# A kernel of sparse attention and two MLPs: the splitting jobs of its first 17 slots dealt out anew

## The reference

```python
scores = scale * np.matmul(q, k.transpose(0, 1, 3, 2))
kth = np.partition(scores, -top_k, axis=-1)[..., -top_k:-top_k + 1]      # top_k = 32
scores = np.where(scores >= kth, scores, -1000000000.0)
attn = softmax(scores)
out = np.matmul(attn, v)
```

```python
h = x @ w_in                                             # MLP 1
g = np.where(h >= 1, h, np.where(h <= -1, 0.0, (h + 1) ** 2 / 4))
x = g @ w_out
h = np.maximum(x @ w_in2, 0.0)                           # MLP 2
out = h * h @ w_out2
```

## Time and profile before

| | us |
|---|---|
| median of 3 runs | 1287.52 (1285.49 to 1288.41) |
| the profiled execution, whole | 1287.39 |
| its span, first to last instruction | 1285.6 |
| PE busy | 1194.8 (93%) |
| DVE busy | 910.6 (71%) |
| POOL busy | 783.9 (61%) |
| ACT busy | 721.8 (56%) |

### The profile page before, as it was taken

One profiled execution on the slowest core, in us unless ns is written; L12 is line 12 of the kernel. 1 busy time (PEld: TensorE's weight loads), 2 busy tenths in 40 slices (PEclk: granted clock), 3 DMA queues, 4 the chain that ended last, 5 costly groups with the idle time before them and its releaser, 6 DMA issues.

```text
span 1285.6 us, 24517 instructions
## 1 busy us (share of the span) xinstructions
PE 1194.8 (93%) x8760; PEld 1132.5 (88%) x8760; DVE 910.6 (71%) x2039; ACT 721.8 (56%) x1617; POOL 783.9 (61%) x637
## 2 busy tenths in 40 slices
PE   2677888999999999999999999999999999999998
PEld 1566878988888999999999999999989999999997
DVE  5789899989899998989999999989861111111121
ACT  4555566766655476776767654556543565643332
POOL 2999787787788776777766767666562222222222
PEclk9966799999999999999999999999999999999999
DMA  5899748565879972543437851445429500780000
GB/s 194 275 341 349 255 164 274 187 232 209 321 254 341 387 300 74 170 166 122 130 114 263 314 197 39 140 151 198 147 77 354 217 34 1 265 325 8 27 17 17
DMA packets 98728, 245.89 MB, mean 191 GB/s; under 512 B 7344, under 2 KB 48304, under 8 KB 86320
## 3 DMA queue, kind: packets, MB, share of 16 engines
q1 hardware_dynamic: 98608, 244.33, 53.7%
HBM read 167.23 MB, written 77.07 MB: 190 GB/s over the span
## 4 chain that ended last, share of the span: by engine, by line
PE 69%; POOL 11%; ACT 8%; DVE 5%; issue 4%; DMA 1%; SPq 0%; ACTq 0%; POOLq 0%
PE h_ps L581 21%; PE y_ps L602 14%; PE y_ps L596 12%; PE pv_ps L540 6%; PE score_ps L581 6%; POOL s_sb L1045 4%; PE tr_ps L513 4%; POOL prob L1050 3%; PE score_ps L478 3%; DVE top L860 2%; DVE rest L862 2%; ACT prob L699 1%; POOL kq_lo L1029 1%; POOL w_out L1037 1%; ACT s_sb L676 1%
## 5 line engine op out<-in xcount | busy, mean ns | idle before, releaser
L1063 POOL TENSOR_TENSOR g_lo<-g_sb,g_hi 128x256 fp32r<-128x256 f32 x288 | 217.2, 754 | 405.1 <-ACT g_hi L778 404.9
L581 PE MATMUL h_ps<-xt_hi,w_in 128*128 128x256 f32 x1880 | 391.3, 291 | 3.5 <-DVE xt_lo L908 2.0
L581 PEld LDWEIGHTS h_ps<-xt_hi,w_in 128*128 128x128 f32 x1880 | 309.6, 191 | 6.7 <-issue 3.0
L860 DVE MAX8 top<-rest 128x8 f32<-128x576 f32 x432 | 303.8, 744 | 0.0
L1045 POOL TENSOR_SCALAR s_sb<-s_sb,top 128x576 f32<-128x576 f32 x144 | 258.4, 1794 | 51.5 <-DVE top L860 50.6
L581 PE MATMUL h_ps<-xt_lo,w_in 128*128 128x256 f32 x940 | 266.2, 283 | 0.0
L596 PE MATMUL y_ps<-g_hi,w_out 128*128 128x256 f32 x1152 | 232.6, 285 | 0.4 <-POOL g_lo L1063 0.3
L778 ACT ACTIVATE g_hi<-g_sb 128x256 fp32r<-128x256 f32 x288 | 121.0, 420 | 184.7 <-DVE g_sb L917 68.8
L862 DVE MATCH_REPLACE8 rest<-top,rest 128x576 f32<-128x576 f32 x288 | 211.4, 741 | 0.0
L602 PE MATMUL y_ps<-w_out,g_hi 128*128 128x512 f32 x576 | 203.3, 394 | 0.3 <-POOL g_lo L1063 0.3
L596 PEld LDWEIGHTS y_ps<-g_hi,w_out 128*128 128x128 f32 x1152 | 190.4, 193 | 1.7 <-POOL g_lo L1063 0.5
(11 more groups left out here) (79 smaller groups left out, 1954.9 us busy)
## 6 DMA issues: line engine op xcount, KB each, us to landing
w_in<-w_scratch SPq DMA_DIRECT2D x32, 1024.0 KB, 6.7
w_out<-w_scratch SPq DMA_DIRECT2D x32, 1024.0 KB, 8.0
ks<-ks_scratch SPq DMA_DIRECT2D x47, 576.0 KB, 5.5
qs<-qs_scratch SPq DMA_DIRECT2D x78, 256.0 KB, 4.4
stage<-in_w_dram SPq DMA_DIRECT2D x32, 512.0 KB, 4.7
w_scratch<-w_in SPq DMA_DIRECT2D x16, 1024.0 KB, 6.8
w_scratch<-w_out SPq DMA_DIRECT2D x16, 1024.0 KB, 8.3
v_sb<-in_vv_dram SPq DMA_DIRECT2D x48, 325.0 KB, 5.5
```

The costliest lines, as they stand in the source:

```text
L581: last = pe.matmul(h_bank(k), wi[:, f // 2, w, m, cols], x[:, m, :], start=(m == 0 and n == 0), stop=(m == KT - 1 and n == 2))
L860: dve.max(best, src[:, :]).then_inc(rank_step, 1)
L1063: pool.tensor_tensor(g_lo[k % 2][:, :], g_sb[k % 2][:, :], g_hi[k % 2][:, :].bitcast(F32), ALU.subtract).then_inc(g_lo_done, 1)
```

## The change

- Jobs in slots 0 to 18: no slot before 14 but slot 0 holds more than one splitting job on POOL. Preps 1 to 8 go from slots 0, 2, 4, 7, 9, 13, 15, 17 to slots 1, 3, 5, 11, 13, 17, 19, 29; preps 9 to 11 go from 28, 30, 32 to 31, 33, 35. Weight blocks 0 to 15 go to the slots of `W1_SLOT`; blocks 12 and 14 are split by DVE, in slots 14 and 15.
- Blocks 0 to 15 have four staging buffers: `xr` and `ys`, which are idle until slot 18, join the two. Three blocks are loaded before slot 0.
- `kq_scratch` holds whole rows of 1216 elements: `restack` has three DMAs (608, 608 and 320 KB) in place of six (two of 288 and four of 320 KB), and `load_qs` has two with pieces of 512 bytes in place of one with pieces of 1024.
- `restack` stands first in SP's slot, ahead of the loads of ks, v and qs.
- `split_first` is cut in two, and DVE ranks the first tiles between its parts; prep 0's subtraction goes from DVE to POOL.
- On DVE the sums of slot n-2 are handled one or two ranking steps later.
- `split_w` on POOL and DVE waits for the lo part of block i-2.

```diff
-PREP_SLOT = (-1, 0, 2, 4, 7, 9, 13, 15, 17, 28, 30, 32, 38, 41, 44, 47)
+PREP_SLOT = (-1, 1, 3, 5, 11, 13, 17, 19, 29, 31, 33, 35, 38, 41, 44, 47)
-W1_PER_SLOT = (1, 2, 1, 2, 1, 2, 1, 1, 1, 1, 1, 1, 1)
+W1_SLOT = [-1, 0, 0, 2, 4, 6, 7, 8, 9, 10, 12, 14, 14, 15, 15, 16]
+STAGE_SLOT = [-1, -1, -1, 0, 1, 2] + [s - 1 for s in W_SLOT[6:]]
...
 def by_vector(i):
-    return i >= WBLOCKS and i % 2 == 1
+    return i in (12, 14) or (i >= WBLOCKS and i % 2 == 1)
+def stage_at(i):
+    return i % 4 if i < WBLOCKS else i % 2
...
-    ks_dram = [scratch(f"ks_scratch{g}", [2, 2 * DIM, SEQ]) for g in range(PREPS)]
-    qs_dram = [scratch(f"qs_scratch{g}", [QT, 2, 2 * DIM, 2, P]) for g in range(PREPS)]
+    kq_dram = [scratch(f"kq_scratch{g}", [3, 2 * DIM, KQ]) for g in range(PREPS)]
...
+        def stage_of(i):
+            return (stage[0], stage[1], xr, ys)[stage_at(i)]
...
                 for x, part in enumerate((kq_hi, kq_lo)):
-                    sp.dma_start(ks_dram[g][x, :, :], part[:, 0:SEQ].bitcast(F32)).then_inc(restacked, 16)
-                    for var in range(2):
-                        sp.dma_start(qs_dram[g][:, x if var == 0 else 1 - x, :, var, :]
-                                     .rearrange("t p n -> p t n"),
-                                     part[:, SEQ:KQ].rearrange("p (t n) -> p t n", t=QT)
-                                     .bitcast(F32)).then_inc(restacked, 16)
+                    sp.dma_start(kq_dram[g][x, :, :], part[:, :].bitcast(F32)).then_inc(restacked, 16)
+                sp.dma_start(kq_dram[g][2, :, SEQ:KQ], kq_hi[:, SEQ:KQ].bitcast(F32)).then_inc(restacked, 16)
...
             def load_qs(g, t, i):
-                sp.dma_start(qs[i][:, :, :, :].bitcast(F32),
-                             qs_dram[g][t].rearrange("x (d h) v n -> (x d) h v n", h=2)).then_inc(qs_loaded[i], 16)
+                cols = slice(SEQ + P * t, SEQ + P * (t + 1))
+                for var in range(2):
+                    sp.dma_start(qs[i][:, :, var, :].bitcast(F32),
+                                 kq_dram[g][var:var + 2, :, cols].rearrange("x (d h) n -> (x d) h n", h=2)
+                                 ).then_inc(qs_loaded[i], 16)
...
             def slot(n):                        # SP
+                if n and n - 1 in PREP_SLOT:
+                    restack(PREP_SLOT.index(n - 1))
                 if n < NORMAL and n % 2 == 0:
                     if n // 2 + 1 < NORMAL // 2:
                         load_slot_ks(n // 2 + 1)
...
-                if n and n - 1 in PREP_SLOT:
-                    restack(PREP_SLOT.index(n - 1))
...
-            stage_block(0)
+            for i in range(3):
+                stage_block(i)
             restack(0)
-            load_kq(1)
...
-            split_first(0)                      # ACT
-            split_first(1)
+            split_first(0, 0)
+            split_first(1, 0)
             copy_scores(0, 0)
+            split_first(0, 1)
             copy_scores(0, 1)
-            split_kq(0)
+            split_first(1, 1)
+            split_new(-1)
...
                 both(0)                         # DVE, slot(n)
+                if n == 0:
+                    split_first(0, 1)
+                    split_first(1, 1)
...
-                if past:
-                    add_to_total(n - 2)
                 both(1)
...
-                if past:
-                    invert_total(n - 2)
-                both(2)
-                if past:
+                behind = 1 if n < UP_POS[0] // 3 else 0
+                for op in (2, 3, 4):
+                    if past and op == 2 + behind:
+                        add_to_total(n - 2)
+                    if past and op == 3 + behind:
+                        invert_total(n - 2)
+                    if op == 4:
+                        if past and not behind:
+                            scale_pv(n - 2)
+                        at(3 * n + 1)
+                    both(op)
+                if past and behind:
                     scale_pv(n - 2)
...
+            split_kq(0)                         # POOL, ahead of slot 0
+            for i in new_blocks(-1):
+                split_w(i)
```

More of the change, by code:

```diff
@@ L221, in build @@
         zeroed = sem("zeroed")
-        w_staged = [sem(f"w_staged{i}") for i in range(2)]
+        w_staged = [sem(f"w_staged{i}") for i in range(4)]
         first_loaded = [sem(f"first_loaded{i}") for i in range(2)]
@@ L646, in _, with split_first @@
         def _(act):
-            def split_first(t):
+            def split_first(t, a):
                 act.wait_ge(first_loaded[t], 16)
[L650 to L655, removed]
+                if a == 0:
+                    act.activation(ks[0][:, t, :], first_k(t), ACT.Copy).then_inc(first_hi, 1)
+                for var in range(2):
+                    rows = slice(DIM * var, DIM * (var + 1))
+                    act.activation(qs[a][rows, t, var, :], first_q(t, a)[rows, :],
+                                   ACT.Copy).then_inc(first_hi, 1)
             def split_kq(g):
@@ L659, in split_kq @@
                 if g:
-                    act.wait_ge(restacked, 16 * 6 * g)
+                    act.wait_ge(restacked, 16 * 3 * g)
                 act.activation(kq_hi[:, :], kq_lo[:, :].bitcast(F32), ACT.Copy).then_inc(kq_hi_done, 1)
@@ L939, in clear_corners, with split_first @@
                         dve.memset(prob[n % 2][rows, col:col + TAIL], 0.0).then_inc(zeroed, 1)
[L941 to L952, removed]
-                    dve.wait_ge(first_hi, 5 * t + 3 + 2 * a)
-                    for var in range(2):
-                        rows = slice(DIM * var, DIM * (var + 1))
-                        dve.tensor_tensor(qs[a][rows, t, 1 - var, :], first_q(t, a)[rows, :],
-                                          qs[a][rows, t, var, :].bitcast(F32),
-                                          ALU.subtract).then_inc(first_lo, 1)
+            def split_first(t, a):
+                if a == 0:
+                    dve.wait_ge(first_hi, 3 * t + 1)
+                    low = slice(DIM, P)
+                    dve.tensor_tensor(ks[0][low, t, :], first_k(t)[low, :], ks[0][low, t, :].bitcast(F32),
+                                      ALU.subtract).then_inc(first_lo, 1)
+                dve.wait_ge(first_hi, 3 * t + 3 if a == 0 else 8 + 2 * t)
+                for var in range(2):
+                    rows = slice(DIM * var, DIM * (var + 1))
+                    dve.tensor_tensor(qs[a][rows, t, 1 - var, :], first_q(t, a)[rows, :],
+                                      qs[a][rows, t, var, :].bitcast(F32),
+                                      ALU.subtract).then_inc(first_lo, 1)
             def split_w(i):
@@ L1014, in slot @@
                     scale_pv(n - 1)
-            split_first(0)
-            split_first(1)
-            split_kq(0)
+            split_first(0, 0)
+            split_first(1, 0)
             for n in range(SLOTS + 2):
@@ L1064, in lo_at, with new_blocks @@
                                        ALU.subtract).then_inc(g_lo_done, 1)
+            def new_blocks(n):
+                return [i for i in range(2 * WBLOCKS) if W_SLOT[i] == n and not by_vector(i)]
             def slot(n):
@@ L1077, in slot @@
                     split_kq(PREP_SLOT.index(n))
-                for i in range(2 * WBLOCKS):
-                    if W_SLOT[i] == n:
-                        split_w(i)
+                for i in new_blocks(n):
+                    split_w(i)
             pool.memset(ident[:, :], 0.0).then_inc(constants_set, 1)
```

44 lines of the change are left out of this document (25 added, 19 removed).

## The result

Forecast 1275.1 us (1268 to 1283). Measured: a median of 1289.61 us over 20 executions (1287.20 to 1295.30), with 1287.28 for the kernel before on the same chips (20 executions, 1285.49 to 1288.98). The ratio is 1.002 (95% interval 1.0012 to 1.0028): no gain, and probably a loss of 0.2%.

A forecast was written before the change was run, and what follows sets the result against it. PE was taken to bound the kernel from about 400 us on, carrying savings in the POOL- and DVE-limited front to the end. A gain of 17.5 less 5.2 is 12.3 from 1287.39: 1275.1 us, range 1268 to 1283.

The forecast's parts named there:

- The start and slots 2 to 9: Earlier first mask, then DVE setting every slot at 10.07 us: slot 10 reached 19.0 us earlier, taken as 17.5.
- rival A: Front bound by data, with slots 3 to 9 longer and the first ks load late: 1284.9 us, chance 0.12.
- Slots 10 to 19: Jobs land where there were none and lengthen the chain: 5.2 us given back, ends 0 and 9.5.
- Slots 20 on: Preps 8 to 11 move later but stay where PE is the limit: counted 0.
- the tail equal, with PE still at 99%: Sign in the late stages that the forecast holds: tail unchanged and PE still busy 99%.
- rival D: Slots 17 to 35: ks comes too late behind the restack, 6.0 us six times: 1311 us, chance 0.07.
- The DMAs: Restacks on SP take 6.3 us, at most 7.6, with one more issue per slot; all hidden, counted 0.
- Rival E: Slots 14 and 15: DVE's two block subtractions are shut out until POOL's end, costing 3.8: 1278.9 us, chance 0.05.
- Rival C: Slots 10 to 19 give everything back because POOL's chain there decides when PE is fed: 1287 us, chance 0.05.

The follow-up runs named there:

- tail_earlier: The changed kernel with preps 8 to 11 one slot earlier, in slots 28, 30, 32 and 34, nothing else: 1282.97 us, ratio 0.9969.
- sums_old: The changed kernel with DVE's sums of slot n-2 back in their old places between the ranking steps: 1295.34 us, ratio 1.0065.
- ks_last: The changed kernel with ks and q loads of slots 30, 32, 34, 36 behind v, stores and reloads, ahead of the kq load: 1283.70 us, ratio 0.9970.
- before_tail: The kernel before with preps 8 to 11 in slots 29, 31, 33, 35 and restack first in SP's slot: 1302.15 us, ratio 1.0121.
- prep_16_18: The changed kernel with preps 6 and 7 in slots 16 and 18, weight block 15 in 17, preps 8 to 11 in 28 to 34: 1280.48 us.
- the last run: The changed kernel with the slots of prep_16_18, blocks 0 to 15 all on POOL, at most one per slot from 10 to 19: 1278.82 us, ratio 0.9928.

## Why the prediction was wrong

*The start and slots 2 to 9: right.* Slot 10 was reached 19.1 us earlier; the sum said 19.0, and 17.5 was taken for caution. The five profiles with this code up to slot 10 have 15.6 to 19.6, with a mean of 17.9, so that this one comes so near to 19.0 is in part luck. POOL's first mask stood at 22.03 (forecast 22), slots 3 to 9 lasted 9.97 each in six of seven cases (forecast 10.07), and DVE was busy throughout. DVE ranked from 8.29. Of rival A (bound by data) this profile shows little: over slots 3 to 9 a DMA share of 0.83 and no wait of DVE; the late kq tile of slot 5 in tail_earlier is of that kind and cost 1.9. Its count against A was too low, though: 253 GB/s were forecast for these slots and 305 measured. sums_old shows that the later sum alone carries 3.4 to 5.8 of the 19.

*Slots 10 to 19: the mechanism right, the size too small.* Forecast 5.2, measured 9.7, just past the upper end of 9.5; in tail_earlier and ks_last, with the same code there, 12.9 and 12.5. Two terms were mis-sized. The two slots with a second block cost 14.38 and 14.40 each, where the sum had 12.57 with 1.0 for both together: DVE and POOL met in both slots (1.0 each on POOL), and ACT's second hi copy, which the sum let pass for nothing, came on top (argued above, not taken apart). And slot 19 lasted 18.01, 4.6 over the 13.39 of before, where 1.4 was taken of 0 to 2.8: besides POOL's 2.79 and 2.60, ACT makes both hi parts ahead of `g_hi`, for which POOL waited 3.93. In return slots 10 to 13 gained 1.1, with slot 11 at full clock (12.98 against 14.44 before).

*Slots 20 on: "They stay where PE is the limit; count 0." This is the step that failed.* It lost 10.1 us between slots 28 and 38. The sign that the prediction named, "the tail equal, with PE still at 99%", did not come: PE was busy 92.61 of 100 us. PE was the limit there only so long as it was fed; the cover was read from PE's busy time, not from the queue that feeds ACT. The prediction named `restack` ahead of the loads and said that everything behind waits, and then priced only one victim, ks (rival D), which no wait of PE in these slots shows late. The rival needed the line "and the kq tile, the q tiles and the stores stand behind ks"; the first of these was late by 3.6 us. before_tail shows that this step costs 14.0 us on the old front, tail_earlier that it makes 8.9 of the 10.1 on the new one, and ks_last that the wait at the head of the queue is the cause.

*The DMAs.* A restack was put at 6.3 us from its first issue to the load behind it, 7.6 at most. It took 5.25 at the start (15.18 to 20.43), but 7.84 in slot 32 (415.29 to 423.13), where two weight reloads of 1024 KB had been issued at 407.24 and 408.62; the medians of such reloads in 400 to 470 are 10.3 and 11.7 us to landing, so they were still under way. "All hidden, 0" was wrong: it was hidden from the reader of ks, not from the queue.

*The account.* For the profiled executions alone, from the forecast to 1288.72: 1275.1, less 1.6 (19.1 for 17.5), plus 4.5 (9.7 for 5.2), plus 10.1 for slots 28 to 37, plus 0.6 for small shifts in slots 20 to 27 and behind 38: 1288.7. It holds for this one execution with its good front and middle.

*Rival E* did not come: DVE's subtraction took 1.68. It also shows the order that no row of before had: DVE began at 173.91, 0.13 after POOL's g_lo (173.78 to 174.50), and took 1.68 where 1.21 is its shortest; POOL's subtraction began at 174.46, with DVE's ending at 175.59, and took 3.39. The Trainium skill, "SBUF — State Buffer", section "Who interferes with whom", has the later of the two wait for the earlier; by that rule POOL would have 1.13 + 2.38 = 3.51 and DVE 0.59 + 1.21 = 1.80 as an estimate, and the trace (3.39 and 1.68) agrees within 0.12. The rival assumed that DVE would meet the long subtraction; it met the short one.

*Rival C's number* (1287) nearly came out, but for another reason than C's: slots 10 to 19 left half of the front's gain, and slots 28 to 37 gave that back. The median lies 0.18% above the kernel before, within the 0.2% that the prediction counted as the same. It had given 0.11 to that and 0.07 to slower, and neither chance covered what happened: C and A have no loss behind slot 20, and D has one with ks as the only victim.

The tail was not all of the miss. With the tail repaired the median is 1282.97 (tail_earlier), which is some 4 of the 12.3 us that were forecast; prep_16_18 has 1280.48, and the last run 1278.82 with the middle spread out as well. What separates the first of these from 1275.1 is the middle, sized too small, and a front that is not as good in every execution as in the profiled one. Left open is why the kq tile of the front, issued at the same distance from the restack, takes some 2 us longer to land in some executions; no run took that apart. The new start was not tried without the rest either.

## What to carry to other kernels

When a step is moved ahead in an in-order issuing queue, list everything behind its wait with its own latest time, and price each one; the thing waited for may be in time while the last in the list is not. A full share of busy time of the bounding engine says that it was fed, not that it will be: look for the load with the least slack. Spread two jobs that share an engine over two slots before counting on a backlog to hide the second: this gave 3.2 us in slots 16 to 19. In slots 14 and 15 it gave 4.0, of which slots 7 to 9, where one of the jobs went, took 2.6 back.

## What the hardware showed that was not expected

In slot 33 PE stood idle for 3.04 us, up to 439.13, and its granted clock fell to 0.50 (1.2 GHz) inside that wait, at 438.26, and was back at 1.00 (2.4 GHz) at 445.08; in the same slot of ks_last, without that wait, it was 1.00 throughout. So a late transfer costs more than its wait. Slots 33 and 34 lasted 33.2 us together, against 27.4 in ks_last, 5.8 more. PE's wait is 3.0 of it, and in the 6.8 us at half clock PE was busy 5.95, half of which, 3.0, is an estimate of what the clock cost. And the clock differs between executions of the same instructions: slot 11 (window, columns as above) in the kernel after and in tail_earlier, in that order.

```profile
125.15:138.13 12.98, 10.94 (x88) 10.24 (x88) 11.62 (x26) 8.06 (x18) 10.60 (x8) 1.00 0.09 37
```

```profile
127.79:142.81 15.02, 13.57 (x97) 13.39 (x97) 11.28 (x26) 7.94 (x18) 10.50 (x8) 0.85 0.07 28
```

The same slot takes 2.0 us more where the clock has a mean of 0.85: in tail_earlier it stood at 0.50 from 125.38 to 132.20, in the kernel after at 1.00 from 117.40 on. And a transfer's landing follows the load: the kq tile of 608 KB landed after 10.2 us in the stretch from 423 to 448, beside 410 to 419 GB/s in the windows above, and another of the same size, issued at 22.42, after 5.1 beside 335 GB/s; a whole restack of 1536 KB at the start, beside 300 GB/s, took 5.25.
